# Forming the differences of the blocks of w_out and w2 on GpSimd instead of VectorE in a three-stage fp32 kernel on one core

## The chip, the core and the metric

The kernel runs on one NeuronCore of a Trainium2 chip. The core has TensorE (PE, matrix multiply), VectorE (DVE), ScalarE (ACT), GpSimd (POOL) and SyncE (SP, which here only issues DMAs). Each engine runs its own program in order and waits on semaphores for the others. The metric is the time of one execution in microseconds; the kernel before takes 1177.3 us, the median of three runs (1177.16 to 1177.48).

## The reference

```python
# 1: chunked attention on q, k, v (4, 8, 576, 64), chunk = 64
scores = scale * np.matmul(q_c, k_c.transpose(0, 1, 2, 4, 3))
attn = softmax(scores);  x = np.matmul(attn, v_c)          # laid out as (2304, 512)
# 2: gated pair: w_a, w_b (512, 1536), w_out (1536, 512)
x = ((x @ w_a) * (x @ w_b)) @ w_out
# 3: four experts: w1 (4, 512, 1024), w2 (4, 1024, 512)
p = domain_probs / (domain_probs.sum(-1, keepdims=True) + 1e-09)
for e in range(4):
    out += p[:, e:e + 1] * (np.maximum(x @ w1[e], 0.0) @ w2[e])
```

## The kernel before, in words

The 2304 tokens are worked in three thirds of 768, T = 0, 1, 2. In each third TensorE runs three stages: the pairs of w_a and w_b (`make_pair`), the product with w_out (`first_x2` for T = 0, `later_x2` after), and eight phases w = 0 to 7 over halves of experts (`first_part` and `second_part` for T = 0, `make_h` and `make_out` after). Every fp32 product is three matmuls on a rounded high part and a low part: ScalarE rounds the high part (a copy to fp32r), VectorE subtracts it from the source to get the low part (helper `rest`, line 1689).

Most products are also done in blocks by a seven-product scheme, which needs differences of blocks of the weights. In the first third, w_out and w2 are multiplied plainly, but their block differences are prepared on the side for the later thirds: formed, split into high and low parts, and stored to DRAM in `kept_wo` and `kept_w2`. That side work is what the change touches:

- `sum_wo(u)`, u = 0, 1, 2, on VectorE (lines 1904 to 1909): four subtractions of 128x512 from the raw blocks in `raw[:, 1]` into `wo_three` and `wo_lone`. It runs inside the w_out stage of T = 0. ScalarE rounds the result (`round_wo_sums`), VectorE forms its low part (`low_wo_sums`), SyncE stores it (`store_wo_sums`). `wo_three` and `wo_lone` are one buffer each, so the sums of u wait until the stores of u - 1 have landed (`wot_kept`). SyncE loads the next raw rows of w_out only after the sums (`wot_sum`).
- `sum_w2(w)`, w = 0 to 7, on VectorE (lines 2010 to 2015): four such subtractions into `three_f` and `lone_f`, in the phases of T = 0. `round_wt` (ScalarE), `low_wt` (VectorE) and the stores to `kept_w2` follow. The sums of w wait until the stores of w - 1 have landed (`wt_kept`), and SyncE loads the next w2 after them (`wt_sum`).

The order on each engine is the order in which the code is written. VectorE and ScalarE therefore hold up everything behind a step that waits: on ScalarE `round_wo_sums(1)` stands ahead of `round_g(6)`, which TensorE needs for its step 6 of 12 in the w_out stage (`gs`, three buffers), and `round_wo_sums(2)` stands ahead of `round_wo(11)` and `round_g(11)`, needed for step 11. `sum_w2(7)` stands at the end of phase 6; ScalarE's `round_wt(7, 0)` is the last thing in its phase 6, ahead of `seed_b` of phase 7, a copy in PSUM that TensorE waits for. In `second_part` TensorE needs the low parts of h (`low_h`, line 2034; C11, C22, C21, C12 in this order, the middle two read from `c2`, printed as c, in SBUF) before it multiplies by w2.

GpSimd does nothing but build an identity matrix at the start.

Of the kernel before, what the change touches and what calls it, by code (L numbers as in the profile page):

```python
# [5 lines left out]
F32 = mybir.dt.float32  # L6
F32R = mybir.dt.float32r
BF16 = mybir.dt.bfloat16
ALU = mybir.AluOpType
# [4 lines left out]
HI, LO = 0, 1  # L14
# [56 lines left out]
def build(nc, q, k, v, wab_in, wo_in, w1_in, w2_in, probs, out, out_t):  # L71
# [5 lines left out]
    with ctx:  # L77
# [117 lines left out]
        def raw_w2(b):  # L195

            return raw[:, 1, b * 512:(b + 1) * 512]
# [8 lines left out]
        def raw_wo_block(kh, col):  # L206

            return raw[:, 1].rearrange("p (t n) -> p t n", t=4)[:, 2 * kh:2 * kh + 2, col * 256:(col + 1) * 256]
# [115 lines left out]
        def set_e(T, w):  # L324
            return pair_no(T, NPAIR) + PH * T + T + w
# [345 lines left out]
        @block.gpsimd  # L671
        def _(pool):
            pool.memset(ident[:, :], 0.0).then_inc(ident_zero, 1)
            pool.wait_ge(ident_zero, 1)
            pool.affine_select(out=ident[:, :], in_=ident[:, :], compare_op=ALU.not_equal, fill=1.0, base=0,
                               pattern=[[-1, P]], channel_multiplier=1).then_inc(ident_set, 1)

        @block.tensor
        def _(pe):
# [1004 lines left out]
        def _(dve):  # L1684
            def f32(ap):
                return ap.bitcast(F32)
# [202 lines left out]
                dve.wait_ge(gs_hi, i + 1)  # L1889
                rest(gs[:, i % 3, :, LO, :], g[:, WO_ORDER[i]], gs[:, i % 3, :, HI, :]).then_inc(gs_lo, 1)  # L1890

            def sum_wo(u):

                def place(c):
                    return f32(wo_three[:, c, :, LO, :] if c < 3 else wo_lone[:, :, LO, :])

                for n in range(4):
                    dve.wait_ge(wo_in_s[n], 16 * (u + 1))
                if u == 0:
                    dve.wait_ge(p3_made, 2 * set_e(0, 0))  # L1900
                else:
                    dve.wait_ge(wot_kept, 64 * u)
                b11, b12, b21, b22 = (raw_wo_block(n // 2, n % 2) for n in range(4))
                dve.tensor_tensor(place(0), b12, b11, ALU.subtract).then_inc(wot_sum, 1)
                dve.tensor_tensor(place(1), b22, b12, ALU.subtract).then_inc(wot_sum, 1)
                dve.wait_ge(wot_sum, 4 * u + 1)
                dve.tensor_tensor(place(2), b22, place(0), ALU.subtract).then_inc(wot_sum, 1)
                dve.wait_ge(wot_sum, 4 * u + 3)
                dve.tensor_tensor(place(3), b21, place(2), ALU.subtract).then_inc(wot_sum, 1)

            def low_wo_sums(u):
                dve.wait_ge(wot_hi, 2 * u + 1)
                rest(wo_three[:, :, :, LO, :], f32(wo_three[:, :, :, LO, :]), wo_three[:, :, :, HI, :]).then_inc(wot_lo, 1)
# [88 lines left out]
                rest(w2[:, LO, 2 * n:2 * n + 2, :].rearrange("p c n -> p (c n)"), raw[:, 1, n * 1024:(n + 1) * 1024],  # L2002
                     w2[:, HI, 2 * n:2 * n + 2, :].rearrange("p c n -> p (c n)")).then_inc(w2_lo, 1)

            def sum_w2(w):

                dve.wait_ge(raw_in[1], 16 * (3 + w + 1))
                if w:
                    dve.wait_ge(wt_kept, 32 * w)
                dve.tensor_tensor(three_f[:, 0, LO, :], raw_w2(2), raw_w2(0), ALU.subtract).then_inc(wt_sum, 1)  # L2010
                dve.tensor_tensor(three_f[:, 1, LO, :], raw_w2(3), raw_w2(2), ALU.subtract).then_inc(wt_sum, 1)
                dve.wait_ge(wt_sum, 4 * w + 1)
                dve.tensor_tensor(three_f[:, 2, LO, :], raw_w2(3), three_f[:, 0, LO, :], ALU.subtract).then_inc(wt_sum, 1)
                dve.wait_ge(wt_sum, 4 * w + 3)
                dve.tensor_tensor(lone_f[:, LO, :], raw_w2(1), three_f[:, 2, LO, :], ALU.subtract).then_inc(wt_sum, 1)

            def low_wt(w, n):
                dve.wait_ge(wt_hi, 2 * w + n + 1)
                if n == 0:
# [51 lines left out]
            def first_phase(w):  # L2071

                Q = set_e(0, w)
                last = w == PH - 1
                t = TILES + w
                if w == 0:
                    finish_x2()
                else:
                    if w <= TILES:
                        normalise(t - 1)  # L2080
                    if last:
                        low_sum(1, XA22)
                        sum_x(1, XS1)
                        low_sum(1, XA11)
                        split_w2(w, 0)
                        split_w2(w, 1)
                    else:
                        split_w2(w, 0)
                        split_w2(w, 1)
                        sum_w2(w)  # L2090
                low_h(w, "C11", 0, ps[:, BA[0], 0:N])
                add_c(Q, "C22", 0)
                low_h(w, "C11", 1, ps[:, BA[1], 0:N])
                add_c(Q, "C22", 1)
                low_h(w, "C22", 0, c2[:, 0, 0, :])
                add_c(Q, "C21", 0)
                low_h(w, "C22", 1, c2[:, 1, 0, :])
                add_c(Q, "C21", 1)
                low_h(w, "C21", 0, c2[:, 0, 1, :])
                low_h(w, "C21", 1, c2[:, 1, 1, :])  # L2100
                if last:
                    sum_x(1, XS3)
                    sum_x(1, XS2)
                    low_sum(1, XA12)
                    sum_x(1, XS4)
                low_h(w, "C12", 0, ps[:, BB[0], 0:N])
                low_h(w, "C12", 1, ps[:, BB[1], 0:N])
                if w < TILES:
                    shift(t, 0)
                if w < PH - 1:  # L2110
                    for n in range(4):
                        sum_w1(w + 1, n)
                else:
                    for n in range(4):
                        sum_ab(1, 0, n)
                add_out(w, 0)
                if not last:
                    split_w1(w + 1, 0)
                else:
                    low_ab(1, 0, 0)  # L2120
                    low_sum(1, XS3)
                if w == 6:
                    low_wt(6, 0)
                    low_wt(6, 1)
                if w == 0:
                    sum_w2(0)
                add_out(w, 1)
                if not last:
                    split_w1(w + 1, 1)
                else:  # L2130
                    low_sum(1, XS2)
                    low_sum(1, XS1)
                add_out(w, 2)
                if not last:
                    split_w1(w + 1, 2)
                else:
                    low_sum(1, XS4)
                    low_ab(1, 0, 1)
                add_out(w, 3)
                if last:  # L2140
                    low_ab(1, 0, 2)
                    low_ab(1, 0, 3)
                if w < 6:
                    low_wt(w, 0)
                if w == 6:
                    sum_w2(7)
                add_out(w, 4)
                if last:
                    low_ab(1, 0, 4)
                    low_ab(1, 0, 5)  # L2150
                    low_ab(1, 0, 6)
                if w < 6:
                    low_wt(w, 1)
                if w == 6:
                    low_wt(7, 0)
                    low_wt(7, 1)
                add_out(w, 5)
# [224 lines left out]
            for T in range(NTH):  # L2382
                for j in range(PLAIN if T == 0 else 0, NPAIR):
                    run_pair(T, j)
                    if T == NTH - 1 and j < 3:
                        fold(j)
                if T:
                    later_x2(T)
                else:
                    sum_wo(0)  # L2390
                    low_wo_sums(0)
                    low_g(3)
                    low_wo(4)
                    low_wo(5)
                    low_g(4)
                    low_wo(6)
                    low_g(5)
                    sum_wo(1)
                    low_wo(7)
                    low_wo_sums(1)  # L2400
                    low_g(6)
                    for n in range(4):
                        sum_w1(0, n)
                    low_g(7)
                    low_wo(8)
                    low_wo(9)
                    low_g(8)
                    low_wo(10)
                    low_g(9)
                    sum_wo(2)  # L2410
                    low_g(10)
                    low_wo_sums(2)
                    low_wo(11)
                    low_g(11)
                    for n in range(3):
                        split_w1(0, n)
                    low_x2(0, A11, xr(0))
                    dve.wait_ge(xraw_set, 2)
                    dve.tensor_tensor(xr(2), xr(0), xr(1), ALU.subtract).then_inc(s_set, 1)
                for w in range(PH):  # L2420
                    if T == 0:
                        first_phase(w)
                    else:
                        later_phase(T, w)
# [47 lines left out]
```

## Time and profile before

| what | value |
|---|---|
| median of three runs | 1177.3 us |
| the profiled execution | 1177.45 us |
| its span, first to last instruction | 1175.7 us |
| TensorE busy | 1167.7 us (99%), granted clock 1.00 |
| VectorE busy | 859.4 us (73%) |
| ScalarE busy | 506.4 us (43%) |
| GpSimd busy | 0.7 us |

The profile is of one execution. Outside its span lie 1.75 us. A row of the timeline gives an instruction's start, how long it took, its engine and line, what it wrote and read, and in brackets how long the engine had been idle and what ended that. Instructions on VectorE overlap slightly: one of 0.68 us is followed by the next 0.60 us after its start. TensorE starts a matmul of 384 columns each 0.17 us, although one shows as 0.33 us.

### The profile page before, as it was taken

The page shows a single profiled execution, that of the slowest core. Times are in us where ns is not written, and L with a number is a line of the kernel's source. Part 1 is how long each engine was busy: PE and PEld are TensorE (multiplying, and loading weights), DVE is VectorE, ACT ScalarE, POOL GpSimd, SP SyncE. Part 2 cuts the span into 40 slices and gives each one's busy share as a digit, 9 for nine tenths or more (in the row PEclk, how much of TensorE's full clock was granted, in tenths as well). Part 3 has the DMA queues.
Part 4 walks back from the last instruction along what each step waited for, and adds up shares of the span by engine and source line. Part 5 has one row for each costly group of instructions (what it writes and reads, how often), then busy time and mean ns, then how long its engine had stood idle before and what let it go on. Part 6 is the DMA issues. An engine that isn't in the chain of part 4 may idle for free.

```text
span 1175.7 us, 18790 instructions
## 1 busy us (share of the span) xinstructions
PE 1167.7 (99%) x7609; PEld 1128.0 (96%) x7609; DVE 859.4 (73%) x1148; ACT 506.4 (43%) x874; POOL 0.7 (0%) x6
## 2 busy tenths in 40 slices
PE   9999999999999999999999999999999999999998
PEld 8999998888999899999999999999999999999998
DVE  6786889888787893367877777797346787777788
ACT  6555464445544542244444434434233533333334
POOL 0000000000000000000000000000000000000000
PEclk9999999999999999999999999999999999999999
DMA  7396885878987699938777777648894877676761
GB/s 271 129 349 237 296 321 219 330 302 332 348 306 271 259 414 357 332 129 328 309 261 250 280 279 273 239 165 286 256 361 162 339 262 263 252 264 250 265 251 75
DMA packets 73162, 319.54 MB, mean 272 GB/s; under 512 B 7340, under 2 KB 13812, under 8 KB 56692
## 3 DMA queue, kind: packets, MB, share of 16 engines
q1 hardware_dynamic: 72644, 317.56, 73.2%
q8 instruction: 60, 0.98, 0.3%
q10 hardware_dynamic: 432, 0.79, 0.2%
q14 instruction: 26, 0.21, 0.0%
HBM read 221.81 MB, written 96.51 MB: 271 GB/s over the span
## 4 chain that ended last, share of the span: by engine, by line
PE 93%; DVE 3%; DMA 2%; ACT 1%; issue 1%; SPq 0%; DVEq 0%; ACTq 0%
PE ps L681 30%; PE ps L683 30%; PE ps L682 30%; DMA kept_w<-w 1%; PE ps L691 1%; PE ps L710 1%; PE ps L699 1%; DMA kept_w<-lone 1%; PE ps L718 0%; PE ps L754 0%; DVE hw L1689 0%; ACT three L1113 0%; ACT hw L1113 0%; SPq L582 0%; DVE h L2034 0%
## 5 line engine op out<-in xcount | busy, mean ns | idle before, releaser
L681 PE MATMUL ps<-x,wab 128*128 128x384 f32 x504 | 169.2, 336 | 0.1
L683 PE MATMUL ps<-x,wab 128*128 128x384 f32 x504 | 168.4, 334 | 0.0
L682 PE MATMUL ps<-x,wab 128*128 128x384 f32 x504 | 168.4, 334 | 0.0
L1113 ACT ACTIVATE hw<-xraw 128x768 fp32r<-128x768 f32 x112 | 94.8, 847 | 158.3 <-DVE xraw L2172 77.2
L1113 ACT ACTIVATE ps<-ps 128x384 f32<-128x384 f32 (+1 forms) x184 | 91.3, 502 | 160.7 <-PE ps L683 157.1
L681 PE MATMUL ps<-hw,w2s 128*128 128x384 f32 x448 | 151.6, 338 | 0.0
L681 PE MATMUL ps<-x,w1s 128*128 128x384 f32 x448 | 151.5, 338 | 0.0
L683 PE MATMUL ps<-x,w1s 128*128 128x384 f32 x448 | 149.8, 334 | 0.0
L683 PE MATMUL ps<-hw,w2s 128*128 128x384 f32 x448 | 149.7, 334 | 0.0
L682 PE MATMUL ps<-x,w1s 128*128 128x384 f32 x448 | 149.7, 334 | 0.0
L682 PE MATMUL ps<-hw,w2s 128*128 128x384 f32 x448 | 149.7, 334 | 0.0
L1689 DVE TENSOR_TENSOR hw<-xraw,hw 128x768 fp32r<-128x768 f32 x112 | 106.9, 954 | 2.3
L681 PEld LDWEIGHTS ps<-x,wab 128*128 128x128 f32 x504 | 94.6, 188 | 0.8 <-DVE c L1803 0.4
L682 PEld LDWEIGHTS ps<-x,wab 128*128 128x128 f32 x504 | 94.6, 188 | 0.0
L683 PEld LDWEIGHTS ps<-x,wab 128*128 128x128 f32 x504 | 94.6, 188 | 0.0
L681 PEld LDWEIGHTS ps<-hw,w2s 128*128 128x128 f32 x448 | 84.1, 188 | 3.8 <-issue 3.4
L681 PEld LDWEIGHTS ps<-x,w1s 128*128 128x128 f32 x448 | 84.1, 188 | 1.5
L682 PEld LDWEIGHTS ps<-x,w1s 128*128 128x128 f32 x448 | 84.1, 188 | 0.0
L682 PEld LDWEIGHTS ps<-hw,w2s 128*128 128x128 f32 x448 | 84.1, 188 | 0.0
L683 PEld LDWEIGHTS ps<-x,w1s 128*128 128x128 f32 x448 | 84.1, 188 | 0.0
L683 PEld LDWEIGHTS ps<-hw,w2s 128*128 128x128 f32 x448 | 84.1, 188 | 0.0
L681 PE MATMUL ps<-w,h 128*128 128x512 f32 x192 | 76.1, 397 | 1.2 <-DVE h L2034 1.1
(203 smaller groups left out, 2257.2 us busy)
## 6 DMA issues: line engine op xcount, KB each, us to landing
wab<-kept_ab SPq DMA_DIRECT2D x70, 512.0 KB, 5.1
w1s<-kept_w SPq DMA_DIRECT2D x32, 1024.0 KB, 6.6
w2s<-kept_w SPq DMA_DIRECT2D x16, 2048.0 KB, 7.5
w1s<-kept_w SPq DMA_DIRECT2D x16, 1536.0 KB, 6.1
w2s<-kept_w SPq DMA_DIRECT2D x16, 1536.0 KB, 6.2
kept_ab<-wab SPq DMA_DIRECT2D x42, 512.0 KB, 5.6
raw<-in_w SPq DMA_DIRECT2D x16, 1024.0 KB, 10.4
kept_w<-w SPq DMA_DIRECT2D x16, 1024.0 KB, 12.9
```

The source lines that it names most:

```text
L681: pe.matmul(dst, stat(HI), mov(HI), start=first, stop=False, skip_group_check=True)
L682: pe.matmul(dst, stat(HI), mov(LO), start=False, stop=False, skip_group_check=True)
L683: return pe.matmul(dst, stat(LO), mov(HI), start=False, stop=last, skip_group_check=True)
L691: last = pe.matmul(ps[BLK * b:BLK * (b + 1), bank + r, n * BLK:(n + 1) * BLK], slot_q(t)[rows, b, n, :], slot_k(t)[rows, b, n, :], start=n ...
L699: last = pe.transpose(ps[:, bank, n * P:(n + 1) * P], slot_p(t)[:, n * P:(n + 1) * P], ident[:, :])
L710: last = pe.matmul(ps[BLK * r:BLK * (r + 1), bank + u, at:at + BLK], slot_v(t)[rows, b, r, m, :], slot_pT(t)[rows, 2 * r + m, BLK * b:BLK ...
L1113: return act.activation(dst, src, ACT.Copy)
L1689: return dve.tensor_tensor(dst, src, f32(hi), ALU.subtract)
```

## The change

The functions `sum_wo` and `sum_w2` move from VectorE's program to GpSimd's, with the same four subtractions and the same semaphores. GpSimd runs them one after the other: three times `sum_wo`, then eight times `sum_w2`. Their calls in VectorE's program go. `sum_w2(0)` gets one wait more (`x2_lo`, the last low part of the second stage's result, because `three_f` lies over a buffer still in use until then).

```diff
+            def sum_wo(u):
+
+                def place(c):
+                    return (wo_three[:, c, :, LO, :] if c < 3 else wo_lone[:, :, LO, :]).bitcast(F32)
+
+                for n in range(4):
+                    pool.wait_ge(wo_in_s[n], 16 * (u + 1))
+                if u == 0:
+                    pool.wait_ge(p3_made, 2 * set_e(0, 0))
+                else:
+                    pool.wait_ge(wot_kept, 64 * u)
+                b11, b12, b21, b22 = (raw_wo_block(n // 2, n % 2) for n in range(4))
+                pool.tensor_tensor(place(0), b12, b11, ALU.subtract).then_inc(wot_sum, 1)
+                pool.tensor_tensor(place(1), b22, b12, ALU.subtract).then_inc(wot_sum, 1)
+                pool.wait_ge(wot_sum, 4 * u + 1)
+                pool.tensor_tensor(place(2), b22, place(0), ALU.subtract).then_inc(wot_sum, 1)
+                pool.wait_ge(wot_sum, 4 * u + 3)
+                pool.tensor_tensor(place(3), b21, place(2), ALU.subtract).then_inc(wot_sum, 1)
+
+            def sum_w2(w):
+
+                pool.wait_ge(raw_in[1], 16 * (3 + w + 1))
+                if w == 0:
+                    pool.wait_ge(x2_lo, x2_count(0, S4))
+                if w:
+                    pool.wait_ge(wt_kept, 32 * w)
+                pool.tensor_tensor(three_f[:, 0, LO, :], raw_w2(2), raw_w2(0), ALU.subtract).then_inc(wt_sum, 1)
...
+            for u in range(3):
+                sum_wo(u)
+            for w in range(PH):
+                sum_w2(w)
@@ first_phase(w) on VectorE
                         split_w2(w, 0)
                         split_w2(w, 1)
-                        sum_w2(w)
...
-                if w == 0:
-                    sum_w2(0)
                 add_out(w, 1)
...
-                if w == 6:
-                    sum_w2(7)
                 add_out(w, 4)
@@ the w_out stage of T = 0 on VectorE
-                    sum_wo(0)
                     low_wo_sums(0)
...
                     low_g(5)
-                    sum_wo(1)
                     low_wo(7)
                     low_wo_sums(1)
                     low_g(6)
...
                     low_g(9)
-                    sum_wo(2)
                     low_g(10)
                     low_wo_sums(2)
```

VectorE's order around `sum_wo(1)`, in the w_out stage of the first third, was this:

```order
L1689 TENSOR_TENSOR gs<-g,gs 128x2x384
L1904 TENSOR_TENSOR wo_three<-raw 128x2x256
L1905 TENSOR_TENSOR wo_three<-raw 128x2x256
L1907 TENSOR_TENSOR wo_three<-raw,wo_three 128x2x256
L1909 TENSOR_TENSOR wo_lone<-raw,wo_three 128x2x256
L1689 TENSOR_TENSOR wo_b<-raw,wo_b 128x2x256
L1689 TENSOR_TENSOR wo_three<-wo_three 128x6x256
L1689 TENSOR_TENSOR wo_lone<-wo_lone 128x2x256
L1689 TENSOR_TENSOR gs<-g,gs 128x2x384
```

and in the changed kernel, where `rest` is line 1727, it is this:

```order
L1727 TENSOR_TENSOR gs<-g,gs 128x2x384
L1727 TENSOR_TENSOR wo_b<-raw,wo_b 128x2x256
L1727 TENSOR_TENSOR wo_three<-wo_three 128x6x256
L1727 TENSOR_TENSOR wo_lone<-wo_lone 128x2x256
L1727 TENSOR_TENSOR gs<-g,gs 128x2x384
```

The low part of `wo_three` and, behind it, the one of `gs` for step 6 now follow sums made on another engine.

At the end of phase 6 of the first third VectorE had the sums of the last w2 between two additions to the output (`acc`):

```order
L1689 TENSOR_TENSOR w<-tsum,w 128x1536
L2050 SCALAR_TENSOR_TENSOR acc<-ps,pw,acc 128x512
L2010 TENSOR_TENSOR three_f<-raw 128x512
L2011 TENSOR_TENSOR three_f<-raw 128x512
L2013 TENSOR_TENSOR three_f<-raw,three_f 128x512
L2015 TENSOR_TENSOR lone_f<-raw,three_f 128x512
L2050 SCALAR_TENSOR_TENSOR acc<-ps,pw,acc 128x512
L1689 TENSOR_TENSOR three<-three_f,three 128x3x512
L1689 TENSOR_TENSOR lone<-lone_f,lone 128x512
```

In the changed kernel the same place reads:

```order
L1727 TENSOR_TENSOR w<-tsum,w 128x1536
L2057 SCALAR_TENSOR_TENSOR acc<-ps,pw,acc 128x512 x2
L1727 TENSOR_TENSOR three<-three_f,three 128x3x512
L1727 TENSOR_TENSOR lone<-lone_f,lone 128x512
L2057 SCALAR_TENSOR_TENSOR acc<-ps,pw,acc 128x512
L1727 TENSOR_TENSOR x<-xf_later,x 128x768
```

The second addition is no longer behind the sums; the low parts of `three` and `lone` still are, now through GpSimd and ScalarE.

GpSimd's program begins, after the identity matrix, with these rows of the first two `sum_wo`:

```order
L690 TENSOR_TENSOR wo_three<-raw 128x2x256
L691 TENSOR_TENSOR wo_three<-raw 128x2x256
L693 TENSOR_TENSOR wo_three<-raw,wo_three 128x2x256
L695 TENSOR_TENSOR wo_lone<-raw,wo_three 128x2x256
L690 TENSOR_TENSOR wo_three<-raw 128x2x256
L691 TENSOR_TENSOR wo_three<-raw 128x2x256
L693 TENSOR_TENSOR wo_three<-raw,wo_three 128x2x256
L695 TENSOR_TENSOR wo_lone<-raw,wo_three 128x2x256
```

There are 44 such instructions in all, and nothing else stands between them.

## Rows read from the trace of the kernel before

**Rows 1.** The page's busy times, and who waited on PE from 20 to 1170 us.

```profile
PE 1167.7 (99%) x7609; PEld 1128.0 (96%) x7609; DVE 859.4 (73%) x1148; ACT 506.4 (43%) x874; POOL 0.7 (0%) x6
...
PE ps L681 <- DVE h L2034: 1.1, 1, 1.1
```

**Rows 2.** Timeline of POOL, whole kernel (start us, us, ...).

```profile
0.24 0.10 POOL L2454 MEMSET const-float32-0.0<- 128x1 f32 x1 [0.24 <-issue]
...
0.73 0.20 POOL L673 MEMSET ident<- 128x128 f32 x1 [0.29 <-POOLq L2454]
1.17 0.29 POOL L675 TENSOR_SCALAR_AFFINE_SELECT ident<-ident 128x128 f32<-128x128 f32 x1 [0.23 <-POOL ident L673]
```

**Rows 3.** Timeline of PE and ACT, first w_out sums.

```profile
116.01 0.33 PE L681 MATMUL ps<-gs,wo_b 128*128 128x384 f32 x1
...
121.44 1.49 ACT L1113 ACTIVATE wo_three<-wo_three 128x1536 fp32r<-128x1536 f32 x1 [5.78 <-DVE wo_lone L1909]
```

**Rows 4.** Timeline of DVE, ACT and PE, second w_out sums to step 6.

```profile
132.40 0.69 DVE L1904 TENSOR_TENSOR wo_three<-raw 128x512 f32<-128x512 f32 x1 [1.84 <-DMA kept_wo<-wo_lone]
...
134.33 0.69 DVE L1909 TENSOR_TENSOR wo_lone<-raw,wo_three 128x512 f32<-128x512 f32 x1
...
138.85 0.95 DVE L1689 TENSOR_TENSOR gs<-g,gs 128x768 fp32r<-128x768 f32 x1
...
135.05 1.49 ACT L1113 ACTIVATE wo_three<-wo_three 128x1536 fp32r<-128x1536 f32 x1 [4.97 <-DVE wo_lone L1909]
...
141.00 0.33 PE L681 MATMUL ps<-gs,wo_b 128*128 128x384 f32 x1
```

**Rows 5.** Timeline of DVE and PE, third w_out sums to step 11.

```profile
147.89 0.69 DVE L1904 TENSOR_TENSOR wo_three<-raw 128x512 f32<-128x512 f32 x1 [0.64 <-DMA kept_wo<-wo_lone]
...
154.95 0.95 DVE L1689 TENSOR_TENSOR gs<-g,gs 128x768 fp32r<-128x768 f32 x1
...
159.72 0.33 PE L681 MATMUL ps<-gs,wo_a 128*128 128x384 f32 x1
```

**Rows 6.** Timeline of DVE and PE, phase 0.

```profile
175.17 1.23 DVE L1689 TENSOR_TENSOR w<-raw,w 128x1024 fp32r<-128x1024 f32 x1
...
178.17 0.55 DVE L2034 SCALAR_TENSOR_TENSOR h<-c,h 128x384 fp32r<-128x384 f32 x1
...
179.10 0.55 DVE L2034 SCALAR_TENSOR_TENSOR h<-c,h 128x384 fp32r<-128x384 f32 x1
...
180.04 1.23 DVE L2034 SCALAR_TENSOR_TENSOR h<-c,h 128x384 fp32r<-128x384 f32 x2
...
181.41 0.47 PE L681 MATMUL ps<-w,h 128*128 128x512 f32 x1
```

**Rows 7.** Timeline of DVE and PE, phase 1.

```profile
205.57 0.69 DVE L2010 TENSOR_TENSOR three_f<-raw 128x512 f32<-128x512 f32 x1 [0.58 <-DMA kept_w<-lone]
...
211.84 1.23 DVE L2034 SCALAR_TENSOR_TENSOR h<-c,h 128x384 fp32r<-128x384 f32 x2
...
213.57 0.47 PE L681 MATMUL ps<-w,h 128*128 128x512 f32 x1
```

**Rows 8.** Timeline of DVE, ACT and PE, end of phase 6 and phase 7.

```profile
393.80 0.69 DVE L2010 TENSOR_TENSOR three_f<-raw 128x512 f32<-128x512 f32 x1 [2.71 <-DMA kept_w<-lone]
...
397.98 1.76 DVE L1689 TENSOR_TENSOR three<-three_f,three 128x1536 fp32r<-128x1536 f32 x1 [0.90 <-ACT three L1113]
...
409.64 1.23 DVE L2034 SCALAR_TENSOR_TENSOR h<-c,h 128x384 fp32r<-128x384 f32 x2
...
396.45 1.49 ACT L1113 ACTIVATE three<-three_f 128x1536 fp32r<-128x1536 f32 x1 [9.16 <-DVE lone_f L2015]
397.85 0.85 ACT L1113 ACTIVATE ps<-ps 128x384 f32<-128x384 f32 x2
...
399.27 0.33 PE L681 MATMUL ps<-x,w 128*128 128x384 f32 x1
...
411.01 0.47 PE L681 MATMUL ps<-w,h 128*128 128x512 f32 x1 [1.07 <-DVE h L2034]
```

More of the change, by code:

```diff
@@ L676, in _ @@
                                pattern=[[-1, P]], channel_multiplier=1).then_inc(ident_set, 1)
+            def sum_wo(u):
[21 more added lines that the diff above has]
+                pool.tensor_tensor(three_f[:, 0, LO, :], raw_w2(2), raw_w2(0), ALU.subtract).then_inc(wt_sum, 1)
+                pool.tensor_tensor(three_f[:, 1, LO, :], raw_w2(3), raw_w2(2), ALU.subtract).then_inc(wt_sum, 1)
+                pool.wait_ge(wt_sum, 4 * w + 1)
+                pool.tensor_tensor(three_f[:, 2, LO, :], raw_w2(3), three_f[:, 0, LO, :], ALU.subtract).then_inc(wt_sum, 1)
+                pool.wait_ge(wt_sum, 4 * w + 3)
+                pool.tensor_tensor(lone_f[:, LO, :], raw_w2(1), three_f[:, 2, LO, :], ALU.subtract).then_inc(wt_sum, 1)
+            for u in range(3):
+                sum_wo(u)
+            for w in range(PH):
+                sum_w2(w)
         @block.tensor
@@ L1890, in low_g @@
                 rest(gs[:, i % 3, :, LO, :], g[:, WO_ORDER[i]], gs[:, i % 3, :, HI, :]).then_inc(gs_lo, 1)
[L1892 to L1909, printed above, removed]
             def low_wo_sums(u):
@@ L2003, in split_w2 @@
                      w2[:, HI, 2 * n:2 * n + 2, :].rearrange("p c n -> p (c n)")).then_inc(w2_lo, 1)
[L2005 to L2015, printed above, removed]
             def low_wt(w, n):
```

## The prediction

> **What bounds the kernel now.** I read the busy times first, then who waited for whom on TensorE, then the timelines of the stretches in which the moved sums lie. TensorE is busy 1167.7 of 1175.7 us, and between 20 and 1170 us the view of waits has one entry for it: 1.1 us, once, for VectorE's h [rows 1]. VectorE is busy 73% and is off the path nearly everywhere. So relief of VectorE can give back about 1.1 us at most, and only if it falls just ahead of that one wait. The question is whether the sums, on a slower engine and beside VectorE, make TensorE wait where it does not now.
>
> **The change, part by part.** VectorE loses 44 subtractions of 128x512. One set of four takes it 2.62 us: from 132.40 to 134.33 + 0.69 = 135.02 [rows 4]. That is 11 x 2.62 = 29 us of busy time off VectorE. None of it stands before a TensorE wait except the set ahead of phase 7. In phase 1, where the sums held VectorE from 205.57 on until a store had landed, TensorE's first product with w2 began at 213.57, 0.5 us after the low part of h was ready (211.84 + 1.23 = 213.07), and did not wait for it: what is gained there is cushion [rows 7].
>
> **What a sum costs on GpSimd.** No row has such an instruction on POOL; I bound it. A MEMSET of one element takes 0.10 us and one of 128 takes 0.20, so a stream of 128 costs 0.10, or 0.8 ns an element; AFFINE_SELECT reads one stream and writes one, 0.29 us, so (0.29 - 0.10) / 128 = 1.5 ns an element [rows 2]. A subtraction reads one stream more: 2.3 ns an element, 512 x 2.3 + 0.1 = 1.27 us. From below: without a price for the second stream, 512 x 1.5 + 0.1 = 0.87 us; and VectorE's own pace, 0.66, is the floor. From above: POOL was idle 0.23 us between an instruction and the one that waits on its semaphore [rows 2]; put on each of the four, that makes 1.5 us each. I take 1.27, since it follows from the nearest rows: 5.1 us for a set, D = 5.1 - 2.6 = 2.5 us later than on VectorE from the same start. The ends are D = 0 (0.9 at 0.87 us) and D = 3.4.
>
> The Trainium skill ("GPSIMD Engine Reference", Performance versus the Vector engine) measures a subtraction-like add of 2048 fp32 elements at 4497 ns on GpSimd and 2293 on VectorE, 1.96 times. By that ratio a set would take 5.1 to 5.4 us; no run here shows it yet, and the sum does not use it.
>
> **Where D falls on the path.**
>
> (A) The w_out stage. First set: it waited for VectorE's turn, while TensorE had already left the pairs at 116.01; ScalarE took up the result at 121.44 [rows 3]. GpSimd can begin at about 116.3, and 116.3 + 5.1 = 121.4: the same, no cost. Second set: VectorE began it at 132.40, when a store landed, so GpSimd begins then too, and ScalarE (134.33 + 0.69, then 135.05) begins D later. Behind it on ScalarE and VectorE stand the rounding, the low parts, and then gs of step 6, ready at 138.85 + 0.95 = 139.80; TensorE starts that step at 141.00 [rows 4]. It starts a waiting product 0.14 us after the low part is ready (409.64 + 1.23 = 410.87, then 411.01) [rows 8], so the slack is 1.06 us, and the stall D - 1.06 = 1.4. Third set: its start waits for the stores of the second (147.89), so it begins D later and ends 2D later; gs of step 11 was ready at 154.95 + 0.95 = 155.90 and is wanted at 159.72 [rows 5]. Slack 3.68, so TensorE is late by 2D - 3.68 = 1.3, and the 1.4 already lost covers that. A = 1.4 us: max(D - 1.06, 2D - 3.68). At the ends of D it is 0 and 3.1.
>
> (B) Phase 0. The sums now run right after the low part that ends the second stage, from about 175.3 on, five us long; VectorE then does the low parts of h, and TensorE takes its first w2 product at 181.41, 0.14 us after the last of C21 (180.04 + 1.23 = 181.27) [rows 6]. There is no slack. Before, the sums came later, with nothing beside them. If the two engines don't disturb each other B = 0. If a sum and a VectorE instruction with two operands in SBUF (h<-c,h at 178.17, 179.10 and 180.04; the ones that read PSUM not) exclude each other, three of these wait on average some 0.8 us for a sum of 1.27 to end: 2.4 us. No row has both engines busy at once, so I take the middle, 1.2.
>
> (C) Phase 7. The last set waits for a store that lands at 393.8; VectorE began at once, and ScalarE took its result at 396.45. From there the chain to TensorE's wait is tight: ScalarE's rounding, the low part at 397.98, and VectorE without a gap worth the name until h is ready at 410.87, when TensorE had already waited 1.07 us [rows 8]. The addition to acc that VectorE can do earlier was hidden under ScalarE's rounding. So this costs D in full: C = 2.5. On the way the seeding of the PSUM bank (ps<-ps from 397.85, the first half done at about 398.3, wanted at 399.27 [rows 8]) comes about 1.5 us too late, but that lies inside the same delay.
>
> Phases 1 to 6: the sums end about 2.5 us after their start later than before, but their users (rounding and low parts near the end of the phase) come ten us after; SyncE's load of the next w2, queued behind `wt_sum`, has most of a phase. VectorE begins its h up to 2.5 us earlier, which covers contention there. I cost it at nothing; without that cover each phase could lose what phase 0 does.
>
> Sum: 1.4 + 1.2 + 2.5 = 5.1 us on the profiled execution's 1177.45, which is 0.15 above the median of the runs; from the median, 1177.3 + 5.1 = **1182.4 us**.
>
> **Rivals.** First, exclusion: B at its full 2.4, and 1.4 + 2.4 + 2.5 = 6.3, so 1183.6 us. For it: each sum reads two operands in SBUF, as does VectorE's h<-c,h, and the slack there is nil [rows 6]. Against it: nothing but that no row shows the two together. The Trainium skill ("SBUF — State Buffer", SBUF: two separate sides) states that rule: the port pair that the two engines share is an exclusive lock for the whole instruction. No trace here can confirm it so far.
>
> Second, on the other side, not slower: GpSimd's sum takes 0.66 to 0.9 us. Then D is 0 to 1.0, the slack of 1.06 us takes up the whole of A, and C is at most 1.0; with B at 0 to 0.5 the time is 1177.3 to 1178.8. It decides from about 0.93 us an instruction downward. For it: 0.87 us by AFFINE_SELECT's pace [rows 2], if the second operand is free. Against it: a second stream has to be read, and MEMSET shows that a stream costs.
>
> Third, slower sets: 1.5 us each, D = 3.4: A becomes 2 x 3.4 - 3.68 = 3.1, since the third set now ends last, C = 3.4, B 1.2 to 3, together 7.7 to 9.5, so 1185.0 to 1186.8. For it: the 0.23 us after a semaphore [rows 2]; against it: only two of four sums wait for another sum.
>
> **How the numbers follow.** Forecast 55% (its own range, 1180.5 to 1183.2), exclusion 25%, as fast as VectorE 13%, slow sets 7%. The range of 8 in 10 reaches from 1179.2, D about 1.3, to 1185.8, and leaves out most of the second rival and the end of the third. A difference under 0.2%, 2.4 us, can't be told from no change. Slower than 1179.7 us: 85%; within 0.2%: 13%, the second rival; faster by 0.2%: 2%, since TensorE's only wait there is to recover is 1.1 us [rows 1].
>
> **What would show it.** The profile after should have 44 POOL subtractions of about 1.27 us; TensorE waiting about 1.4 us ahead of step 6 of the w_out stage for gs; a wait ahead of the first w2 product of phase 0 that grows with each overlap on VectorE, whose h<-c,h then start late; about 1.5 us ahead of the third block product of phase 7 for ScalarE's seed, and together some 3.6 us up to the first w2 product there, instead of 1.07. VectorE's busy time should fall to about 830 us. The prediction is wrong if the sums are under 0.9 us, if TensorE waits in phases 1 to 6, or if stores land so much earlier that the last set begins well before its turn.

## The result, and the profile after

The changed kernel takes 1185.4 us (median of four runs, 1183.77 to 1186.08) against 1177.4 us for the kernel before on the same chip (1177.16 to 1177.53). The ratio is 1.0065, with an interval of 1.0053 to 1.0078. It is slower by 8.0 us where 5.1 were forecast: inside the range of 1179.2 to 1185.8, near its end. The profiled execution took 1184.99 us, with a span of 1183.2 against 1175.7, so 7.5 us of span are to be found.

The busy times of the kernel after, from its page, which answer to the first of [rows 1]:

```profile
PE 1169.7 (99%) x7609; PEld 1128.8 (95%) x7609; DVE 841.9 (71%) x1104; ACT 505.4 (43%) x874; POOL 63.8 (5%) x50
```

Who waited on TensorE from 20 to 1170 us, from its view of waits (us in total, times, longest), which answers to the second:

```profile
PE ps L719 <- DVE h L2041: 3.2, 2, 1.6
PE ps L719 <- DVE gs L1727: 2.0, 1, 2.0
PE ps L719 <- ACT ps L1151: 1.2, 1, 1.2
```

One wait of 1.1 us has become four, of 6.4 us. VectorE lost 44 instructions and only 17.5 us of busy time. Added up, they took 30.2 us, but they overlap their neighbours slightly: VectorE's other instructions alone kept it busy for 832.4 us in the kernel before. In the kernel after they take 841.9, so they became 9.5 us longer.

The timeline of GpSimd: the first set of w_out's sums, first and last of the second, first of phase 0's, first and last of phase 7's.

```profile
115.93 1.67 POOL L690 TENSOR_TENSOR wo_three<-raw 128x512 f32<-128x512 f32 x1 [114.46 <-PE ps L721]
117.57 1.60 POOL L691 TENSOR_TENSOR wo_three<-raw 128x512 f32<-128x512 f32 x1
119.13 1.28 POOL L693 TENSOR_TENSOR wo_three<-raw,wo_three 128x512 f32<-128x512 f32 x1
120.50 1.29 POOL L695 TENSOR_TENSOR wo_lone<-raw,wo_three 128x512 f32<-128x512 f32 x1
...
132.63 1.29 POOL L690 TENSOR_TENSOR wo_three<-raw 128x512 f32<-128x512 f32 x1 [10.85 <-DMA kept_wo<-wo_lone]
...
136.49 1.28 POOL L695 TENSOR_TENSOR wo_lone<-raw,wo_three 128x512 f32<-128x512 f32 x1
...
178.70 2.22 POOL L704 TENSOR_TENSOR three_f<-raw 128x512 f32<-128x512 f32 x1 [22.64 <-DVE x L1727]
...
398.80 1.29 POOL L704 TENSOR_TENSOR three_f<-raw 128x512 f32<-128x512 f32 x1 [18.86 <-DMA kept_w<-lone]
...
402.67 1.29 POOL L709 TENSOR_TENSOR lone_f<-raw,three_f 128x512 f32<-128x512 f32 x1
```

A sum alone takes 1.29 us (1.27 was taken), and an undisturbed set 5.14 or 5.16. A sum that begins while VectorE works on two operands in SBUF takes up to 2.22.

The timeline of ScalarE, VectorE and TensorE up to step 6 of the w_out stage, which answers to [rows 4]:

```profile
137.81 1.49 ACT L1151 ACTIVATE wo_three<-wo_three 128x1536 fp32r<-128x1536 f32 x1 [8.16 <-POOL wo_lone L695]
...
141.60 0.95 DVE L1727 TENSOR_TENSOR gs<-g,gs 128x768 fp32r<-128x768 f32 x1
...
142.70 0.41 PE L719 MATMUL ps<-gs,wo_b 128*128 128x384 f32 x1 [1.98 <-DVE gs L1727]
```

TensorE stood idle 1.98 us. Counted from start to start, less one matmul's 0.17, it lost 2.14. Behind that wait comes something that no step of the prediction has. The view by windows of the kernel after (window in us; busy us and count of PE, PEld, DVE, ACT, POOL; PE's granted clock; DMA share; GB/s):

```profile
143.00:144.00 1.00, 1.00 (x7) 1.00 (x6) 0.96 (x3) 0.58 (x2) 0.00 (x0) 0.92 1.06 420
144.00:146.00 2.00, 2.00 (x7) 2.00 (x7) 2.00 (x4) 0.00 (x0) 0.00 (x0) 0.50 1.02 420
146.00:148.00 2.00, 2.00 (x9) 2.00 (x9) 2.00 (x4) 0.00 (x0) 0.00 (x0) 0.69 1.03 420
...
150.00:152.00 2.00, 2.00 (x14) 2.00 (x12) 1.70 (x1) 0.00 (x0) 2.00 (x2) 1.00 1.01 360
```

From about 143.8 to 147.2 us TensorE ran at a granted clock of 0.50, the lower of its two levels (1.2 GHz of 2.4); before the wait it had been busy without a break at 1.00. Seven matmuls in 2 us stand where there are else twice as many. From the start of step 6 to that of step 7 it took 5.83 us (142.70 to 148.53) where before it took 4.16 (141.00 to 145.16): 1.67 us.

The timeline of VectorE and TensorE in phase 0, which answers to [rows 6]:

```profile
178.54 1.23 DVE L1727 TENSOR_TENSOR w<-raw,w 128x1024 fp32r<-128x1024 f32 x1
...
181.54 1.05 DVE L2041 SCALAR_TENSOR_TENSOR h<-c,h 128x384 fp32r<-128x384 f32 x1
182.51 0.55 DVE L1844 TENSOR_TENSOR c<-ps,t_sb 128x384 f32<-128x384 f32 x1
182.98 1.18 DVE L2041 SCALAR_TENSOR_TENSOR h<-c,h 128x384 fp32r<-128x384 f32 x1
...
184.55 1.62 DVE L2041 SCALAR_TENSOR_TENSOR h<-c,h 128x384 fp32r<-128x384 f32 x2
...
186.32 0.47 PE L719 MATMUL ps<-w,h 128*128 128x512 f32 x1 [1.64 <-DVE h L2041]
```

The instructions that read PSUM keep their 0.55 us. Those that read c and h, both in SBUF, went from 0.55 to 1.05 and 1.18, and the pair from 1.23 to 1.62: 1.5 us in all. An instruction that had begun ahead of the sum kept its time: w<-raw,w, which reads two operands in SBUF too, began 0.16 us before the sum at 178.70 and took its 1.23, and it was the sum that took 2.22, 0.93 more than alone.

The timeline of ScalarE, VectorE and TensorE in phases 6 and 7, which answers to [rows 8]:

```profile
378.86 1.49 DVE L2041 SCALAR_TENSOR_TENSOR h<-c,h 128x384 fp32r<-128x384 f32 x1
...
403.99 1.48 ACT L1151 ACTIVATE three<-three_f 128x1536 fp32r<-128x1536 f32 x1 [11.81 <-POOL lone_f L709]
405.38 0.85 ACT L1151 ACTIVATE ps<-ps 128x384 f32<-128x384 f32 x2
...
405.91 0.44 PE L719 MATMUL ps<-x,w 128*128 128x384 f32 x1 [1.25 <-ACT ps L1151]
...
418.55 0.47 PE L719 MATMUL ps<-w,h 128*128 128x512 f32 x1 [1.55 <-DVE h L2041]
```

Phase 7 has both of its waits: 1.25 for ScalarE's seed, then 1.55 for h where it was 1.07. In phase 6 one h<-c,h took 1.49 us. It began 0.22 us after a GpSimd sum (378.64) that took 1.30, and it made TensorE 0.32 late. Phases 1 to 5 have such an h<-c,h each, and there TensorE was not late.

The account, each entry from start to start less the usual distance and less what the kernel before has in that place:

| place | us |
|---|---|
| wait ahead of step 6 | 2.14 |
| step 6 at half clock | 1.67 |
| phase 0, 1.81 - 0.27 | 1.54 |
| phase 6 | 0.32 |
| phase 7, 1.41 + 0.15 + 1.77 - 1.29 | 2.04 |
| w_out stage begun earlier, 115.59 instead of 116.01 | -0.42 |
| together | 7.3 of 7.5 |

### The profile page after: what moved, and what is told of

Its sections match the earlier page's. It is cut to its first block, busy times and chain, and to the rows that moved or that the text cites. A ratio compares the mean times of both kernels' runs of the same rounds, so it can differ in the third digit from the quotient of the medians.

```text
span 1183.2 us, 18791 instructions
## 1 busy us (share of the span) xinstructions
PE 1169.7 (99%) x7609; PEld 1128.8 (95%) x7609; DVE 841.9 (71%) x1104; ACT 505.4 (43%) x874; POOL 63.8 (5%) x50
## 4 chain that ended last, share of the span: by engine, by line
PE 89%; DVE 5%; ACT 2%; DMA 1%; POOL 1%; issue 1%; SPq 0%; POOLq 0%; DVEq 0%
PE ps L719 29%; PE ps L720 29%; PE ps L721 29%; DVE h L2041 1%; PE ps L748 1%; PE ps L729 1%; PE ps L737 1%; DMA kept_w<-lone 1%; DVE x L1727 0%; DMA kept_wo<-wo_lone 0%; PE ps L792 0%; DMA early<-in_q 0%; DVE hw L1727 0%; DVE wo_three L1727 0%; DVE c L1841 0%
```

## The experiments

Each kernel was measured beside the kernel before on the same chip, and ratios have 95% intervals. "Gap" below is TensorE's loss from start to start, as in the table. The first four separate the places; the next four ask for the mechanism in phase 0 and for the price of the last set; the last four try other orders and combine what was learned.

**e1, the w_out sums alone** (the w2 sums back on VectorE).

```diff
             for u in range(3):
                 sum_wo(u)
-            for w in range(PH):
-                sum_w2(w)
```

> Only the three w_out sets on GpSimd, the w2 sets on VectorE as before. Theory of places: TensorE pays at step 6 of the w_out stage alone: a wait of 2.1 us for gs, then about 3.4 us at the 0.5 clock, which cost 1.7; less the 0.4 by which this span's stage started early. About 1181.0 us. Rival, a price per GpSimd instruction wherever it stands (8.0 / 44 = 0.18 us): 12 x 0.18 = 2.2, so 1179.6 us.

It took 1180.37 us (1179.12 to 1181.52) against 1177.56, ratio 1.0024 (1.0015 to 1.0033): +2.8. From its timeline:

```profile
143.19 0.41 PE L717 MATMUL ps<-gs,wo_b 128*128 128x384 f32 x1 [2.19 <-DVE gs L1725]
```

And from its windows:

```profile
144.00:146.00 2.00, 2.00 (x13) 2.00 (x12) 2.00 (x4) 0.06 (x1) 0.00 (x0) 1.00 1.04 422
```

The wait is even longer than in the kernel after, a gap of 2.35, and the clock did not fall in this execution: step 7 came 4.24 us later. So such a wait does not bring the fall each time, and the stage's loss without it is the wait alone. The other executions of e1 were not traced beyond their mean granted clock, but that tells something: four of the ten have 0.998, as the traced one of the kernel after, and took 1180.88 to 1181.52 us; the other six have 0.999 or 1.000 and took 1179.12 to 1180.62. The four are 1.5 us longer on average, near the 1.67 that the fall cost above. Whether the fall comes seems to vary between executions of one kernel.

**e2, the w2 sums alone** (the w_out sums back on VectorE).

```diff
-            for u in range(3):
-                sum_wo(u)
             for w in range(PH):
                 sum_w2(w)
```

> Only the eight w2 sets on GpSimd, the w_out sets on VectorE as before. Theory of places: phase 0 waits 1.5 us more (h<-c,h on VectorE stretched), phase 6 0.3, phase 7 2.0: 3.9 us, 1181.3 us, and no stretch at the 0.5 clock. Rival, a price per instruction: 32 x 0.18 = 5.8, so 1183.2 us.

1181.48 us (1180.96 to 1182.14), ratio 1.0033 (1.0021 to 1.0046): +3.9. Its gaps are 1.82 in phase 0, 0.32 in phase 6 and 0.69, 0.18 and 1.77 in phase 7. Phase 0's is that of the kernel after, so it has nothing to do with the w_out sums. The two halves of the change together give 2.8 + 3.9 = 6.7 of 8.0 us. The 2.8 is the median of executions of which four in ten seem to have the fall; these four, at 1181.3 on average, lie 3.7 above the kernel before, and 3.7 + 3.9 = 7.6 is an estimate of the sum with a fall in it. All four executions of the kernel after have a mean clock of 0.998 or 0.999, four of e2's five one of 1.000.

**e3, the w2 sums of phases 1 to 6 alone.**

```diff
-            for u in range(3):
-                sum_wo(u)
-            for w in range(PH):
+            for w in (1, 2, 3, 4, 5, 6):
                 sum_w2(w)
```

> Only the w2 sets of phases 1 to 6 on GpSimd; w_out's, phase 0's and phase 7's on VectorE as before. Theory of places: 0.3 us in phase 6 (there h<-c,h stretched by a sum eats a slack of 0.25 us), nothing else: 1177.7 us. Rival, a price per instruction: 24 x 0.18 = 4.4, so 1181.8 us. If relief of VectorE were worth something it would be under 1177.4.

1177.12 us (1176.60 to 1178.03), ratio 0.9997 (0.9988 to 1.0006): no difference. TensorE lost 0.32 in phase 6 and had it back in phase 7, whose gap was 0.93 instead of 1.29. From its view of waits:

```profile
PE ps L717 <- DVE h L2070: 0.7, 1, 0.7
```

These six of the eleven sets are free, and bring nothing either. That rules out the rival of these first runs, a price for each sum wherever it stands, which would have cost 4.4 us here.

**e4, TensorE busy during the wait at step 6.** The kernel after, with 38 small matmuls of the tile `warm` ahead of step 6. They also overwrite partial sums in that bank.

```diff
                 for i in range(FA - 2):
+                    if i == 6:
+                        for _ in range(38):
+                            pe.matmul(ps[:, 1, 384:512], warm[:, 0:P], warm[:, 0:P], start=True, stop=True,
+                                      skip_group_check=True)
```

> The changed kernel, with 38 matmuls of 128 columns on zeros into unused columns of PSUM in the place where TensorE waits ahead of step 6 of the w_out stage. Theory: the clock falls because TensorE stood still there for 2.1 us; kept busy, it stays at its full level, step 6 takes 4.2 us instead of 5.8, and the time is about 1.7 us less than the changed kernel's, 1183.7 us. Rival: the clock falls for another reason (power, or GpSimd's running): it falls anyway and the time stays at 1185.4 us or grows by what the added matmuls outlast the wait.

1188.23 us (1185.73 to 1188.30), ratio 1.0082 (1.0069 to 1.0096). The expectation missed. From its timeline:

```profile
141.03 2.30 PE L872 MATMUL ps<-warm 128*128 128x128 bf16 x38
...
143.48 0.41 PE L719 MATMUL ps<-gs,wo_b 128*128 128x384 f32 x1 [0.16 <-DVE gs L1731]
```

And from its windows:

```profile
144.00:146.00 2.00, 2.00 (x14) 2.00 (x13) 2.00 (x4) 0.35 (x1) 0.00 (x0) 1.00 1.06 419
...
188.00:190.00 2.00, 2.00 (x6) 1.52 (x6) 1.97 (x4) 0.00 (x0) 0.00 (x0) 0.50 1.09 445
...
409.20:412.40 3.20, 3.20 (x11) 3.20 (x11) 3.20 (x4) 3.20 (x6) 0.00 (x0) 0.50 0.30 123
```

Step 6 ran at full clock, as expected. But the same 3.4 us at 0.50 now came twice elsewhere: after the wait in phase 0 (gap 1.88) and after the one in phase 7 (gap 2.83). Both waits are in the kernel after too, the second only half as long (1.41), and had no fall behind them in its profiled run. So the fall is a second cost that such a wait can have, and which wait has it differs between the traces. Whether filling a wait prevents it, this run can't show, since e1's wait had no fall without any filling.

**e5, phase 0's sums behind h** (the w2 sums alone, phase 0's set held until VectorE has finished h).

```diff
                 if w == 0:
-                    pool.wait_ge(x2_lo, x2_count(0, S4))
+                    pool.wait_ge(h_lo, h_count(0, "C12", 1))
```

> Only the w2 sets on GpSimd, and the one of phase 0 held back until the last low part of h (C12) of that phase is made. Theory of exclusion: the 1.5 us of phase 0 are VectorE's h<-c,h (both operands in SBUF) shut out by the sums; with the sums behind them they take 0.55 us again, TensorE waits 0.3 us there as before, and the time is 1181.5 - 1.5 = 1180.0 us. Rival: phase 0 is late because VectorE or ScalarE enters it late; then the wait stays at 1.8 us and the time at 1181.5.

1180.53 us (1180.16 to 1180.89) against 1176.97, ratio 1.0028 (1.0017 to 1.0039). Phase 0's gap is back at 0.28. From VectorE's timeline:

```profile
178.03 0.55 DVE L2058 SCALAR_TENSOR_TENSOR h<-c,h 128x384 fp32r<-128x384 f32 x1
...
184.10 1.67 DVE L2024 TENSOR_TENSOR tsum<-raw,tsum 128x512 f32<-128x512 f32 x1
...
187.39 1.78 DVE L2029 TENSOR_TENSOR tsum<-raw,tsum 128x512 f32<-128x512 f32 x1
```

h<-c,h takes 0.55 again, and VectorE's own sums that now lie beside GpSimd's take 1.7 instead of 0.7. The 1.5 us won in phase 0 were mostly not kept: phase 1 has a gap of 0.31 and the seed's wait in phase 7 is 1.38 instead of 0.69. That is +3.6 us where the w2 sums without this edit gave +3.9, and the two intervals overlap.

**e6, the last set back on VectorE** (w2 sums of phases 0 to 6 on GpSimd, 7 on VectorE).

```diff
-            for w in range(PH):
+            for w in (0, 1, 2, 3, 4, 5, 6):
                 sum_w2(w)
```

> The w2 sets of phases 0 to 6 on GpSimd, the one of phase 7 on VectorE as before. Theory: the last set costs what a GpSimd set is longer than a VectorE set, 5.2 - 2.6 us, less what the landing store gives back; TensorE's waits at the third block of phase 7 (0.7) and before its first w2 product (1.8) go back to none and about 1.0, so 1181.5 - 1.5 to 2.0 = 1179.5 to 1180.0 us. Rival: phase 7 is late because of the sums in phase 6 before it; then it stays at 1181.5.

1179.13 us (1178.44 to 1179.27), ratio 1.0015 (1.0007 to 1.0024). Phase 7's only gap is 0.38, against 0.69 + 0.18 + 1.77 = 2.64 with that set on GpSimd. By these gaps the last set costs 2.3 us in its place, close to D = 2.5. By the medians of e2 and e6, which were measured on different chips, it is 3.9 - 2.2 = 1.7.

**e7, subtractions that belong to nothing, on GpSimd in phase 0.** The kernel before, with five subtractions of 128x384 in a spare buffer where phase 0's sums would run. SyncE uses that buffer only after them.

```diff
+            pool.memset(pb[:, :], 1.0).then_inc(spare_set, 1)
+            pool.wait_ge(x2_lo, x2_count(0, S4))
+            for n in range(5):
+                pool.wait_ge(spare_set, n + 1)
+                pool.tensor_tensor(pb[:, N:2 * N], pb[:, 0:N], pb[:, 0:N], ALU.subtract).then_inc(spare_set, 1)
```

> The kernel before, and on GpSimd five subtractions of 128x384 that nobody uses, one after the other, from the same moment as the changed kernel's sums of phase 0; both operands and the result lie in pb, which is idle then. Theory of exclusion: VectorE's h<-c,h of phase 0 take 1.0 us or more instead of 0.55, its instructions that read PSUM stay at 0.55, TensorE waits about 1.5 us more, 1177.5 + 1.5 = 1179.0 us. Rival, data dependence only (the sums' users late): nobody uses these, so 1177.5 us.

**e8, MEMSETs in the same place**, twelve of 128x384, which write SBUF and read nothing.

```diff
+            for n in range(12):
+                pool.wait_ge(spare_set, n + 1)
+                pool.memset(pb[:, N:2 * N], 0.0).then_inc(spare_set, 1)
```

> The kernel before, and on GpSimd twelve MEMSETs of 128x384 into pb that nobody uses, from the same moment, about as long in total. Theory: only GpSimd's reading of SBUF shuts VectorE's two-operand instructions out, so these cost nothing, 1177.5 us. Rival: any GpSimd instruction that touches SBUF does it, since one port pair carries reads and writes; then h<-c,h are stretched here too, by up to half a microsecond each, and the time is 1178 to 1179 us.

1177.86 us (1177.14 to 1178.37), ratio 1.0008 (0.9998 to 1.0017), with the subtractions, and 1177.28 (1176.50 to 1178.24), ratio 1.0002 (0.9993 to 1.0011), with the MEMSETs. The times can't tell the two apart, and the 1179.0 us expected with the subtractions was too high; the gap in phase 0 can, 1.02 us against 0.28. From the timeline with the subtractions:

```profile
174.72 5.82 POOL L684 TENSOR_TENSOR pb<-pb 128x384 f32<-128x384 f32 x5 [172.57 <-DVE x L1697]
...
177.62 1.13 DVE L2042 SCALAR_TENSOR_TENSOR h<-c,h 128x384 fp32r<-128x384 f32 x1
178.68 0.55 DVE L1814 TENSOR_TENSOR c<-ps,t_sb 128x384 f32<-128x384 f32 x1
179.14 0.71 DVE L2042 SCALAR_TENSOR_TENSOR h<-c,h 128x384 fp32r<-128x384 f32 x1
...
181.62 0.47 PE L689 MATMUL ps<-w,h 128*128 128x512 f32 x1 [0.85 <-DVE h L2042]
```

And from the timeline with the MEMSETs:

```profile
175.06 5.67 POOL L684 MEMSET pb<- 128x384 f32 x12 [172.92 <-DVE x L1697]
...
177.99 0.56 DVE L2042 SCALAR_TENSOR_TENSOR h<-c,h 128x384 fp32r<-128x384 f32 x1
...
178.93 0.55 DVE L2042 SCALAR_TENSOR_TENSOR h<-c,h 128x384 fp32r<-128x384 f32 x1
```

With GpSimd equally busy, h<-c,h is delayed only where GpSimd reads SBUF, and c<-ps,t_sb, which reads PSUM, in neither. The loss comes both ways: the probe's subtractions took 0.83 us at the shortest and 1.81 at the longest. That is the exclusion of the first rival. In the kernel after, too, whichever of the two began first kept its time and the other took about the rest of it longer (phase 0's first sum, phase 6's h<-c,h). The Trainium skill ("SBUF — State Buffer", SBUF: two separate sides) states it as an exclusive lock on a port pair that the two engines share; the traces agree with it.

**e9, the gs of steps 6 and 11 ahead of the sums' rounding** (the w_out sums alone, with the order changed on ScalarE and VectorE; `round_wo(11)` and `low_wo(11)` likewise).

```diff
-                    round_wo_sums(1)
                     round_g(6)
+                    round_wo_sums(1)
...
-                    low_wo_sums(1)
                     low_g(6)
+                    low_wo_sums(1)
```

> Only the w_out sets on GpSimd, and on ScalarE and VectorE the rounding and low parts of gs 6, and of w_out row 11 and gs 11, stand ahead of those of the sums. Theory: the 2.35 us wait at step 6 came from what is queued behind the sums, so it goes, step 11 is on time, and the time is that of before, 1177.2 us, against 1180.4 for the same kernel without the new order. Rival: the w_out stage is late because of the loads that wait for wot_sum (the next raw rows, w2): then a wait stays at step 8 or in phase 0, and the time is 1179 us or more.

1179.79 us (1178.33 to 1181.18) against 1177.34, ratio 1.0021 (1.0011 to 1.0031). The expectation missed. From the timeline of TensorE and VectorE:

```profile
140.74 1.76 DVE L1725 TENSOR_TENSOR wo_three<-wo_three 128x1536 fp32r<-128x1536 f32 x1 [5.32 <-ACT wo_three L1149]
140.76 0.33 PE L717 MATMUL ps<-gs,wo_b 128*128 128x384 f32 x1
...
145.55 0.95 DVE L1725 TENSOR_TENSOR gs<-g,gs 128x768 fp32r<-128x768 f32 x1
...
146.64 0.41 PE L717 MATMUL ps<-gs,wo_b 128*128 128x384 f32 x1 [1.56 <-DVE gs L1725]
```

Step 6 is in time, and step 7 waits 1.56 us: its gs stands in VectorE's order behind the sums' low parts and the sums of w1. The lateness passed one step on, and phase 0's products with x came another 0.64 us late, a wait that e1 does not have.

**e10, the middle sets on GpSimd, and h ahead in phase 7.** The idea was to remove phase 7's wait by moving VectorE's work on x behind all of h; and for comparison **e11, that order alone**, in the kernel before. Both have this edit:

```diff
                     if last:
-                        low_sum(1, XA22)
-                        sum_x(1, XS1)
-                        low_sum(1, XA11)
...
                 low_h(w, "C21", 1, c2[:, 1, 1, :])
+                low_h(w, "C12", 0, ps[:, BB[0], 0:N])
+                low_h(w, "C12", 1, ps[:, BB[1], 0:N])
                 if last:
+                    low_sum(1, XA22)
+                    sum_x(1, XS1)
+                    low_sum(1, XA11)
```

> The w2 sets of phases 1 to 6 on GpSimd as in the third experiment, and in phase 7 VectorE makes its h first and the x sums for the next third after it. Theory: TensorE's wait before the first w2 product of phase 7 (0.9 us) goes, nothing else grows: 1176.3 us. Rival: the x sums are then late for additions to acc or for the next third's pair, and the time is 1177.2 us or more.

> The kernel before with that new order of phase 7 alone, all sums on VectorE. Theory: its wait of 1.3 us goes, 1177.2 - 1.2 = 1176.0 us, so GpSimd's part in the version before this one is worth nothing. Rival: VectorE, with the sums, is then too full for it, and it stays at 1177.2 us.

1180.82 us (1179.82 to 1181.28), ratio 1.0029 (1.0017 to 1.0041), and 1179.69 (1179.47 to 1180.63), ratio 1.0023 (1.0014 to 1.0032). Both expectations missed. Phase 7's gap fell to 0.37 and 0.63, and a new one opened behind it. From the timeline of TensorE in the first of the two:

```profile
437.14 0.44 PE L717 MATMUL ps<-x,wab 128*128 128x384 f32 x1 [2.52 <-ACT ps L1149]
```

And from its windows:

```profile
438.00:440.00 2.00, 2.00 (x8) 2.00 (x7) 1.58 (x3) 1.43 (x4) 0.00 (x0) 0.50 1.02 406
```

And from the timeline of the second:

```profile
437.69 0.44 PE L681 MATMUL ps<-x,wab 128*128 128x384 f32 x1 [2.44 <-ACT ps L1113]
```

From start to start the gaps are 2.69 and 2.61. So it is the order itself that makes the next third's first pair late, with or without GpSimd's help. The clock fell behind the first gap, again for 3.4 us, and not behind the second, of nearly the same length and in the same place. The fall cost 1.7 us there, and e10's two executions at a mean clock of 1.000 took 1179.82 and 1179.92 us where the four below it took 1180.69 to 1181.28.

**e12, what had been tried in the single places, together:** the new order in the w_out stage, phase 0's set behind h, sets 1 to 6 on GpSimd, the last on VectorE.

```diff
                 if w == 0:
-                    pool.wait_ge(x2_lo, x2_count(0, S4))
+                    pool.wait_ge(h_lo, h_count(0, "C12", 1))
...
-            for w in range(PH):
+            for w in range(7):
                 sum_w2(w)
```

> All sets on GpSimd but the last (w2 of phase 7, on VectorE), with the order of the w_out stage as in the first kernel of this group and the w2 set of phase 0 behind that phase's h. Theory: the 8 us of the change lay in these places and their order alone, so what is left is 0.3 us in phase 6: 1177.5 us, with 40 sums on GpSimd. Rival, a price of the sums wherever they are: 1179 us or more.

1180.60 us (1180.08 to 1181.51), ratio 1.0030 (1.0018 to 1.0041). From its view of waits:

```profile
PE ps L719 <- DVE gs L1727: 0.9, 1, 0.9
PE ps L719 <- DVE x L1727: 0.5, 1, 0.5
PE ps L719 <- DVE h L2053: 0.5, 2, 0.3
```

The expectation missed by 3.1 us. The time is as its rival, a price for the sums wherever they are, would have it, but e3's 24 sums had none, and the trace has the loss in places: step 7 waits 1.05 us, phase 0's products with x 0.64, and the products with w2 in phases 0, 1 and 6 0.2 to 0.3 each more than before, while phase 7's wait is 0.9 shorter. After phase 7 TensorE is 2.3 us behind; the interval of the time is 2.1 to 4.8.

No version beats the kernel before. The one with the middle sets alone is level with it.

## Why the prediction was right, point by point

**Direction, places and range: right.** The kernel is slower, through waits ahead of step 6, in phase 0 and in phase 7, as said. That the time lies in the range is in part luck: the sum came out 2.9 us too low and lacked an item of 1.7 us, which the range, laid out for other values of D and B, happened to cover.

**GpSimd's pace: right.** 1.29 us for 1.27, from a scale built on a MEMSET and an AFFINE_SELECT. That disposes of the second and the third rival. How well the scale itself holds is less certain: for 384 elements it gives 0.97, and the undisturbed subtractions of e7, whose two operands are the same data, took 0.83. So part of the match at 512 may be luck. Against VectorE's 0.685 it is 1.88 times, and 5.14 for a set instead of 2.62 makes D = 2.5, as predicted. The Trainium skill ("GPSIMD Engine Reference", Performance versus the Vector engine) has 1.96 times for a longer add; the trace here is a little below that.

**(A), forecast 1.4, measured 2.1 as a wait.** The step that failed is the sentence that the first set costs nothing. It began on time (115.93), but its first two sums took 1.67 and 1.60, beside VectorE's work on wo_a and g. It ended at 121.79, and ScalarE could take it up some 0.4 us later than in [rows 3], 0.8 later counted from the start of the stage. The second set waits for the first one's stores, and so began 0.65 us later, counted in the same way: 132.63 - 115.59 = 17.04 against 132.40 - 116.01 = 16.39 [rows 3, 4]. Its 5.14 us then put ScalarE's rounding at 137.81, 3.2 us later than in [rows 4] after allowing for the stage's earlier start, and 3.2 - 1.06 = 2.1 is the wait. The form of the term, delay less slack, held; the delay was D plus what contention had added to the set before. The third set cost nothing of its own, as the prediction had it: gs of step 11 was ready 5.55 us later than before (160.50 + 0.95 against 155.90), and TensorE had lost 3.4 us by then. Run e1 has the same wait (2.35) without any w2 sums.

**Not foreseen: the fall of the clock, 1.7 us.** It is the largest item that the sum lacks. A wait of 2 us was priced at 2 us. In the profiled run of the kernel after it cost 2.1 and then 1.7 more at half clock. The traced execution of e1 had such a wait without the fall, e4 had two falls after other waits, and e10 had one where e11 had none after nearly the same wait. What decides it stays open. Nor is it shown that the remaining difference, 8.0 against the 6.7 of the two halves apart, is made of such falls. The mean clocks of the executions speak for it (with e1's four low ones the halves give 7.6), but the interval of the kernel after, 6.2 to 9.2 us, holds the 6.7 as well.

**(B), taken at 1.2, measured 1.54.** The middle was taken between nothing and 2.4 because no trace showed both engines busy. The mechanism of the first rival is what happens, shown by e7 against e8 and by e5, but its size was too high: three h<-c,h were stretched, as said, by 0.50, 0.63 and 0.60 us and not by 0.8 each, and 0.2 of it fell into an idle moment ahead of the fourth. Each found a sum already under way, and none waited for a whole one.

**(C), forecast 2.5, measured 2.04.** The last set costs 2.3 by the gaps where it is the only difference (e2 against e6). In the whole kernel part of it is given back; that TensorE already comes late through the waits ahead is my reading, and no run isolates it. Both of the waits named in the prediction are there: 1.25 us for the seed (about 1.5 was said) and 1.55 for h, together 3.3 as gaps where 3.6 were forecast.

**Phases 1 to 6: nearly right.** e3 shows that they cost nothing in the time. One of the prediction's own signs of being wrong, a wait in phases 1 to 6, did appear, 0.32 us in phase 6. And the reason given, that VectorE begins its h up to 2.5 us earlier, was wrong in phase 6, where TensorE was 0.32 late: h<-c,h waits for TensorE's products, so relief of VectorE cannot bring it forward much, and one of 1.49 us beside a sum was enough. The loss comes back only because phase 7 has a wait that absorbs it.

**VectorE's busy time, forecast about 830, measured 841.9.** The prediction took off the 44 instructions, and without them VectorE would be busy 832.4; it put in nothing for stretching, and 9.5 of 27.0 us came back as longer instructions.

## What to carry to other kernels

Work moved to GpSimd beside a busy VectorE should be priced three times: its own longer time where somebody waits for the result, the stretching of every VectorE instruction with two SBUF operands that begins while a GpSimd instruction runs, and the same stretching of a GpSimd instruction that begins while such a VectorE instruction runs, which also delays the sets that follow through their stores. It is free only where nobody waits for many us on either side (here the six middle sets), and there it brought nothing, because VectorE was not the bound. Count a wait of about 2 us on a full TensorE as possibly costing nearly twice its length, and don't expect to remove a late result by reordering its consumers in a full in-order queue: with both orders that were tried the wait turned up further on, at the next step or in the next stage.

## What the runs showed of the hardware that was not expected

- After a loss of 2.14, 1.88, 2.83 and 2.69 us in an otherwise unbroken stream, TensorE ran 3.4 us at a granted clock of 0.50 (the kernel after once, e4 twice, e10 once); after one of 2.35 in e1 and one of 2.61 in e11 it did not.
- Contention between GpSimd and VectorE is mutual and spares PSUM readers: in the kernel after VectorE's h<-c,h went from 0.55 up to 1.49 us and GpSimd's sums from 1.29 up to 2.22, in e5 VectorE's sums from 0.7 up to 1.78. c<-ps,t_sb stayed at 0.55, and beside GpSimd's MEMSETs h<-c,h did too.
- The one that began first kept its time: all seven w<-raw,w that lie beside a sum in the kernel after began ahead of it and took 1.22 or 1.23, while these sums took 1.89 to 2.22.
